# Moving the low parts of activations and weights from VectorE to GpSimd in a two-layer feed-forward

## The chip, the cores and the metric

The kernel runs on one core of one Trainium2 chip. The metric is the device time of one execution in microseconds (us). TensorE has two clock levels here, 1.2 and 2.4 GHz, and the profile records which one was granted.

## The reference, cut to what matters

A delta-rule attention (batch 4, 8 heads, 768 steps, head size 48) makes x of 3072 tokens by 384 features. Two feed-forward layers follow:

```
_moe_ref:  h = x @ w_in                              # 384 -> 2048
           P = a[0] + a[1]*h + a[2]*h^2 + a[3]*h^3
           Q = 1.0 + |b[0]|*|h| + |b[1]|*h^2
           g = P / (Q + 1e-06)                       # the rational layer, layer 0
           x = g @ w_out                             # 2048 -> 384
_moe2_ref: h = x @ w_in;  sp = log(1 + exp(h));  g = h * tanh(sp)   # layer 1
           out = g @ w_out
```

## The kernel before

**Stages.** `delta_rule` runs first, in six tiles of 512 tokens (T = 6, TOK = 512). Its GpSimd program inverts small triangular matrices (lines 224 and 227, tiles `inv_t` and `inv_x`), while VectorE keeps the recurrence going. Then `feed_forward` runs layer 0 over six tiles and layer 1 over six tiles. In its original form GpSimd has no program in `feed_forward`.

**Products in three parts.** A float32 product is made of three fp32r matmuls: high x high, high x low, low x high. So each operand is kept as a high part (a rounded copy, made by ScalarE) and a low part (the operand minus its high part, made by VectorE). Tokens: `x_raw` to `x_hi` (line 918) and `x_lo` (line 1041). Weights: `w_raw` to `w_hi` (line 83) and `w_lo` (line 87). Each such part of x or of one weight pair has 128x1536 elements. Two parities of `x_hi` and `x_lo` and two buffers of `w_raw` exist; `x_raw` is single, and its next load waits for `x_lo_ready`. The load of weight pair n waits until the low part of pair n - 2 is made.

**Blocks.** The 2048 hidden features are cut into 8 pairs of 128 (NP = 8). One block is one pair of one tile: 18 matmuls into `h_ps`, the elementwise function on 128x1024 elements, and 18 matmuls into `o_ps`. `two_tiles` covers 16 blocks (DT = 16), so each layer has 48. TensorE issues the first product of block n + 2 and then the second product of block n. ScalarE's order in a layer-0 block is: square, abs and linear term of block n + 1 (885 to 887), `g_hi` of block n (895), logarithm and exponential of block n + 1 (906, 914), which give the reciprocal. VectorE's order is

```
1018 ratio      val <- val, rec        1026 corrected  den <- den, rec
1031 corrected  val <- den, val         991 below      den <- sq, den
1037 low_part   g_lo <- val, g_hi       997 above      pa  <- pa, h_ps
 999 above      val <- pa, h_ps
```

Lines 997 and 999 read one tile in SBUF and one in PSUM; the other five read two tiles in SBUF. Layer 1 has six VectorE operations in a block: 1020, 1004 (a clip with one input), 1028, 1031, 1010 (reads `h_ps`) and 1037.

**Where the low parts stand.** Splits of x are written into the order by hand. ScalarE makes `x_hi` behind its work of n = 2 and n = 10, and VectorE makes `x_lo` behind its work of n = 3 and n = 11, that is, behind line 999 of that block. The lists LATE and SWAP place the weights: LATE names pairs 4 to 7 of layer 0, in its first blocks; SWAP names the eight pairs of layer 1 (numbers 8 to 15), in the last blocks of layer 0 and the first ones of layer 1. ScalarE makes `w_hi` at the end of the block before the one in which VectorE makes `w_lo`. Pairs 0 to 3 are prepared within `delta_rule`.

Of the kernel before, what the change touches and what calls it, by code (L numbers as in the profile page):

```python
# [5 lines left out]
F32 = mybir.dt.float32  # L6
F32R = mybir.dt.float32r
ALU = mybir.AluOpType
# [7 lines left out]
T = S // (C * CT)  # L16
# [13 lines left out]
NP = FT // 2  # L30
# [8 lines left out]
LATE = [(0, i, i - NP // 2 + 1) for i in range(NP // 2, NP)]  # L39
SWAP = [(1, i, NP + 3 + i) for i in range(NP)]  # L40
# [696 lines left out]
def feed_forward(nc, x1, x2, w1, w2, coef, out, w, hand):  # L737
# [3 lines left out]
    with ExitStack() as ctx:  # L741
        def sb(name, shape, dt=F32):
            return ctx.enter_context(nc.sbuf_tensor(name, shape, dt))

        def sem(name):
            return ctx.enter_context(nc.semaphore(name))

        x_raw = hand.x_raw
        x_hi = sb("x_hi", [P, 2, KT, TOK], F32R)
        x_lo = sb("x_lo", [P, 2, KT, TOK], F32R)  # L750
# [15 lines left out]
        x_hi_ready, x_lo_ready = sem("x_hi_ready"), sem("x_lo_ready")  # L766
# [12 lines left out]
        DT = 2 * NP  # L779
        block = ctx.enter_context(nc.Block())  # L780

        def features(t):
            return t.rearrange("(k p) n -> p k n", p=P)

        @block.sync
        def _(sp):
            def load_x(src, t, tile):

                sp.wait_ge(x_lo_ready, tile)
                hand.load_x(sp, src, t)  # L790

            def store(dst, t, tile):
                sp.wait_ge(o_copied, tile + 2)
                sp.dma_start(features(dst[:, t]), o_stage).then_inc(o_stored, 16)

            sp.dma_start(cf[:, 0:6], coef).then_inc(coef_loaded, 16)

            for cp in range(2):
                sp.wait_ge(hand.y_stored[cp], 32 * T + 32)
            load_x(x1, 1, 1)  # L800
            for i in range(NP // 2 + 2, NP):
                w.load(sp, w1, i)
            with sp.Fori(0, T - 2) as t:
                store(x2, t, t)
                load_x(x1, t + 2, t + 2)
            store(x2, T - 2, T - 2)

            sp.wait_ge(o_stored, 16 * 2)
            load_x(x2, 0, T)
            for i in range(NP):  # L810
                w.load(sp, w2, NP + i)
            store(x2, T - 1, T - 1)
            sp.wait_ge(o_stored, 16 * (T + 1))
            load_x(x2, 1, T + 1)
            with sp.Fori(0, T - 2) as t:
                store(out, t, t + T)
                load_x(x2, t + 2, t + T + 2)
            store(out, T - 2, 2 * T - 2)
            store(out, T - 1, 2 * T - 1)
            sp.wait_ge(o_stored, 16 * (2 * T + 1))  # L820
# [56 lines left out]
        def _(act):  # L877
# [48 lines left out]
            def copy_out(tile):  # L926

                act.wait_ge(g_used, NP * tile + NP + 2)

                act.wait_ge(o_stored, 16 * tile + 16)  # L930
                act_fn(o_stage, o_ps[:], ACT.Copy).then_inc(o_copied, 1)  # L931
# [48 lines left out]
            two_tiles(1, T - 1, None)  # L980
            copy_out(2 * T - 1)

        @block.vector
        def _(dve):
            dve_tt, dve_stt = nc.vector.tensor_tensor, nc.vector.scalar_tensor_tensor

            def below(dt, n):

                e = n % 2
                dve.wait_ge(abs_ready, DT * dt + n + 1)  # L990
                dve_stt(den[:, e], sq[:, e], cf[:, 6:7], den[:, e], ALU.mult, ALU.add).then_inc(q_ready, 1)  # L991

            def above(dt, n):

                e = n % 2
                dve.wait_ge(lead_ready, DT * dt + n + 1)
                dve_tt(pa[:, e], pa[:, e], h_ps[e][:], ALU.mult).then_inc(inner_ready, 1)  # L997
                dve.wait_ge(inner_ready, DT * dt + n + 1)
                dve_stt(val[:, e], pa[:, e], cf[:, 1:2], h_ps[e][:], ALU.add, ALU.mult).then_inc(h_read, 1)  # L999

            def clipped(dt, n):
                e = n % 2
                dve.wait_ge(exp_ready, DT * dt + n - NL1 + 1)
                nc.vector.tensor_scalar(den[:, e], den[:, e], EXP20, None, ALU.min).then_inc(clip_ready, 1)

            def mish_above(dt, n):

                e = n % 2
                dve.wait_ge(one_ready, DT * dt + n - NL1 + 1)
                dve_stt(val[:, e], sq[:, e], -1.0, h_ps[e][:], ALU.add, ALU.mult).then_inc(h_read, 1)  # L1010

            def ratio(layer, dt, n):

                e = n % 2
                dve.wait_ge(rec_ready, DT * dt + n + 1)
                dve.wait_ge(h_read, DT * dt + n + 1 + 2)
                if layer == 0:
                    dve_stt(val[:, e], val[:, e], cf[:, 0:1], rec[:, e], ALU.add, ALU.mult).then_inc(ratio_ready, 1)  # L1018
                else:
                    dve_tt(val[:, e], val[:, e], rec[:, e], ALU.mult).then_inc(ratio_ready, 1)  # L1020

            def corrected(layer, dt, n):

                e = n % 2
                if layer == 0:
                    dve_stt(den[:, e], den[:, e], ONE, rec[:, e], ALU.add, ALU.mult).then_inc(unit_ready, 1)  # L1026
                else:
                    dve_stt(den[:, e], sq[:, e], 1.0, rec[:, e], ALU.add, ALU.mult).then_inc(unit_ready, 1)
                dve.wait_ge(ratio_ready, DT * dt + n + 1)
                dve.wait_ge(unit_ready, DT * dt + n + 1)  # L1030
                dve_stt(val[:, e], den[:, e], 2.0, val[:, e], ALU.subtract, ALU.mult).then_inc(g_ready, 1)  # L1031

            def low_part(dt, n):

                e = n % 2
                dve.wait_ge(g_hi_ready, DT * dt + n + 1)
                dve_stt(g_lo[:, e], val[:, e], -1.0, g_hi[:, e].bitcast(F32), ALU.mult, ALU.subtract).then_inc(g_lo_ready, 1)  # L1037

            def split(tile, par):
                dve.wait_ge(x_hi_ready, tile + 1)  # L1040
                dve_tt(x_lo[:, par], x_raw[:], x_hi[:, par].bitcast(F32), ALU.subtract).then_inc(x_lo_ready, 1)

            def two_tiles(layer, dt, after, splits=()):

                for n in range(DT):
                    following = layer if n + 1 < DT else after
                    ratio(layer, dt, n)
                    if following == 1:
                        clipped(dt, n + 1)
                    corrected(layer, dt, n)  # L1050
                    if following == 0:
                        below(dt, n + 1)
                        low_part(dt, n)
                        above(dt, n + 1)
                    elif following == 1:
                        mish_above(dt, n + 1)
                        low_part(dt, n)
                    else:
                        low_part(dt, n)
                    if n == 3:  # L1060
                        split(2 * dt + 1, 1)
                    if n == NP + 3 and after is not None:
                        split(2 * dt + 2, 0)
                    for l, i, at in splits:
                        if at == n:
                            w.split_lo(nc, dve, NP * l + i)

            dve.sem_inc(g_used, 2)
            dve.sem_inc(h_read, 2)
            nc.vector.memset(shifts[:, 0:1], ONE)  # L1070
            nc.vector.memset(shifts[:, 1:2], 1.0).then_inc(coef_made, 1)
            split(0, 0)
            dve.wait_ge(coef_made, 2)
            below(0, 0)
            above(0, 0)
            two_tiles(0, 0, 0, LATE)
            with dve.Fori(1, T // 2 - 1) as dt:
                two_tiles(0, dt, 0)
            two_tiles(0, T // 2 - 1, 1, [x for x in SWAP if x[2] < DT])
            two_tiles(1, T // 2, 1, [(l, i, n - DT) for l, i, n in SWAP if n >= DT])  # L1080
            with dve.Fori(T // 2 + 1, T - 1) as dt:
                two_tiles(1, dt, 1)
            two_tiles(1, T - 1, None)
# [49 lines left out]
```

## Time and profile before

| what | value |
|---|---|
| median of 3 runs | 1302.22 us (1290.46 to 1315.64) |
| the profiled execution, time | 1274.1 us |
| its span, first to last instruction | 1272.0 us |
| mean granted TensorE clock | 0.932 |
| busy: PE, DVE, ACT, POOL | 1148.9, 932.5, 740.7, 194.8 us |

The profile calls TensorE PE, VectorE DVE, ScalarE ACT and GpSimd POOL. Its times are microseconds from the start of the span. The profiled execution lies below the three timed ones, so sums are made within its span and then carried over to the median as a difference.

### The profile page before, as it was taken

How to read it: one execution, taken by the hardware profiler on the slowest of the kernel's cores; microseconds unless marked ns; L12 is line 12 of the kernel's file. 1: busy time of each engine (PE TensorE's matmuls, PEld its weight loads, DVE VectorE, ACT ScalarE, POOL GpSimd, SP SyncE). 2: the span in 40 equal slices, each digit the busy share in tenths (PEclk: the TensorE clock that was granted, in tenths of full speed). 3: DMA queues.
4: the chain of work that ended last, by engine and by line, in shares of the span. 5: the costliest groups of instructions: out<-in, count | busy, mean ns of one | idle time of the engine just before them, and what ended most of it. 6: DMA issues, size and time to landing. Idle time of an engine off the chain costs nothing.

```text
span 1272.0 us, 23564 instructions
## 1 busy us (share of the span) xinstructions
PE 1148.9 (90%) x9612; PEld 885.4 (70%) x9612; DVE 932.5 (73%) x1042; ACT 740.7 (58%) x932; POOL 194.8 (15%) x365
## 2 busy tenths in 40 slices
PE   6169797979999888999999999988999999999997
PEld 3147474657666666777878777776888888888885
DVE  2733343434444599999999999999978787878885
ACT  1123242424343676777777786878776666667664
POOL 1508655565810000000000000000000000000000
PEclk7569797959899999999999999999999999999999
DMA  6985665645371210101010010223010100001000
GB/s 143 197 166 119 141 142 151 133 111 143 77 206 41 62 50 1 50 1 50 0 46 4 0 50 1 99 67 107 26 50 1 46 4 26 24 12 38 1 26 25
DMA packets 81694, 83.82 MB, mean 66 GB/s; under 512 B 55040, under 2 KB 62720, under 8 KB 81024
## 3 DMA queue, kind: packets, MB, share of 16 engines
q1 hardware_dynamic: 70880, 60.43, 19.0%
q10 hardware_dynamic: 10720, 22.03, 6.3%
q8 instruction: 73, 1.20, 0.4%
q14 instruction: 21, 0.17, 0.0%
HBM read 61.99 MB, written 20.45 MB: 65 GB/s over the span
## 4 chain that ended last, share of the span: by engine, by line
PE 34%; DVE 25%; ACT 4%; issue 3%; DMA 0%; DVEq 0%; ACTq 0%
PE o_ps L825 6%; PE o_ps L826 6%; PE o_ps L827 6%; PE h_ps L825 5%; PE h_ps L827 5%; PE h_ps L826 5%; DVE val L999 4%; DVE val L1018 4%; DVE val L1031 4%; DVE g_lo L1037 3%; DVE den L991 3%; DVE den L1026 3%; DVE pa L997 3%; ACT stage L931 1%; ACT den L886 1%
## 5 line engine op out<-in xcount | busy, mean ns | idle before, releaser
L895 ACT ACTIVATE g_hi<-val 128x1024 fp32r<-128x1024 f32 x96 | 102.0, 1062 | 89.5 <-DVE val L1031 83.7
L825 PE MATMUL o_ps<-g_hi,w_hi_early 128*128 128x512 f32 x288 | 116.6, 405 | 17.8 <-ACT stage L931 14.2
L681 DVE TENSOR_TENSOR u_blk<-hz_ps,w_blk 128x768 f32<-128x768 f32 x48 | 46.0, 957 | 115.5 <-PE hz_ps L390 115.5
L825 PE MATMUL o_ps<-g_hi,w_hi_late 128*128 128x512 f32 x288 | 115.6, 401 | 15.6 <-DVE g_lo L1037 15.6
L1031 DVE SCALAR_TENSOR_TENSOR val<-den,val 128x1024 f32<-128x1024 f32 x96 | 117.7, 1226 | 10.7 <-DVE den L1026 0.5
L525 ACT ACTIVATE stage<-y_ps 128x256 f32<-128x256 f32 x48 | 18.2, 380 | 178.9 <-PE y_ps L422 178.5
L1037 DVE SCALAR_TENSOR_TENSOR g_lo<-val,g_hi 128x1024 fp32r<-128x1024 f32 x96 | 117.6, 1225 | 3.7 <-ACT g_hi L895 3.4
L826 PE MATMUL o_ps<-g_lo,w_hi_early 128*128 128x512 f32 x288 | 115.2, 400 | 0.0
L825 PE MATMUL h_ps<-x_hi,w_hi_early 128*128 128x512 f32 x288 | 113.0, 392 | 2.4 <-DVE val L999 2.0
L827 PE MATMUL o_ps<-g_hi,w_lo_early 128*128 128x512 f32 x288 | 115.0, 399 | 0.0
L825 PE MATMUL h_ps<-x_hi,w_hi_late 128*128 128x512 f32 x288 | 112.5, 391 | 1.6 <-DVE w_lo_late L87 1.6
L826 PE MATMUL o_ps<-g_lo,w_hi_late 128*128 128x512 f32 x288 | 113.0, 392 | 0.0
L827 PE MATMUL o_ps<-g_hi,w_lo_late 128*128 128x512 f32 x288 | 112.8, 392 | 0.0
L826 PE MATMUL h_ps<-x_lo,w_hi_early 128*128 128x512 f32 x288 | 112.8, 392 | 0.0
L827 PE MATMUL h_ps<-x_hi,w_lo_early 128*128 128x512 f32 x288 | 112.6, 391 | 0.0
L826 PE MATMUL h_ps<-x_lo,w_hi_late 128*128 128x512 f32 x288 | 112.1, 389 | 0.0
L827 PE MATMUL h_ps<-x_hi,w_lo_late 128*128 128x512 f32 x288 | 112.1, 389 | 0.0
L367 PE MATMUL warm_ps<-eye 128*128 128x512 bf16 x348 | 110.8, 417 | 0.0
L914 ACT ACTIVATE rec<-rec 128x1024 f32<-128x1024 f32 x96 | 101.0, 1052 | 1.5
L227 POOL TENSOR_TENSOR inv_x<-inv_x,inv_t 128x112 f32<-128x112 f32 (+18 forms) x177 | 97.1, 549 | 13.9
L224 POOL TENSOR_TENSOR inv_t<-inv_n,inv_x 128x112 f32<-128x112 f32 (+18 forms) x177 | 87.7, 496 | 64.2 <-DMA inv_n<-n_dram 50.8
L889 ACT ACTIVATE den<-h_ps 128x1024 f32<-128x1024 f32 x48 | 49.3, 1026 | 67.2 <-PE h_ps L827 67.2
(96 smaller groups left out, 2367.0 us busy)
## 6 DMA issues: line engine op xcount, KB each, us to landing
w_raw<-w SPq DMA_DIRECT2D x14, 768.0 KB, 4.3
kq_gram<-kq_t SPq DMA_DIRECT2D x12, 768.0 KB, 11.1
x_raw<-x_dram SPq DMA_DIRECT2D x12, 768.0 KB, 5.6
kq_run<-kq_t ACTq DMA_DIRECT2D x40, 192.0 KB, 4.0
kv_run<-kv_n ACTq DMA_DIRECT2D x20, 384.0 KB, 5.4
k_norm<-kv_n SPq DMA_DIRECT2D x6, 768.0 KB, 4.9
x_dram<-stage ACTq DMA_DIRECT2D x24, 192.0 KB, 5.1
x_dram<-stage SPq DMA_DIRECT2D x6, 768.0 KB, 4.1
```

The lines of the kernel that those rows point to most:

```text
L224: tt(inv_t[:, 0:r, c], inv_n[:, 0:r, r:r + 1].broadcast_to(shape), inv_x[:, r:r + 1, c].broadcast_to(shape), ALU.mult).then_inc(step, 1)
L227: tt(inv_x[:, 0:r, c], inv_x[:, 0:r, c], inv_t[:, 0:r, c], ALU.subtract).then_inc(step, 1)
L367: nc.tensor.matmul(warm_ps[:], operand[:, 0:P], operand, start=True, stop=True)
L825: nc.tensor.matmul(dst, hi, rhs_hi, start=first, stop=False)
L826: nc.tensor.matmul(dst, hi, rhs_lo, start=False, stop=False)
L827: return nc.tensor.matmul(dst, lo, rhs_hi, start=False, stop=last)
L895: act_fn(g_hi[:, n % 2], val[:, n % 2], ACT.Copy, scale=-1.0).then_inc(g_hi_ready, 1)
L914: act_fn(rec[:, e], rec[:, e], ACT.Exp, scale=-1.0).then_inc(rec_ready, 1)
L999: dve_stt(val[:, e], pa[:, e], cf[:, 1:2], h_ps[e][:], ALU.add, ALU.mult).then_inc(h_read, 1)
L1018: dve_stt(val[:, e], val[:, e], cf[:, 0:1], rec[:, e], ALU.add, ALU.mult).then_inc(ratio_ready, 1)
L1031: dve_stt(val[:, e], den[:, e], 2.0, val[:, e], ALU.subtract, ALU.mult).then_inc(g_ready, 1)
L1037: dve_stt(g_lo[:, e], val[:, e], -1.0, g_hi[:, e].bitcast(F32), ALU.mult, ALU.subtract).then_inc(g_lo_ready, 1)
```

## The change

GpSimd gets a program in `feed_forward`. It makes `x_lo` of tiles 1 to 6 (all of layer 0 but the first tile, and the first tile of layer 1) and `w_lo` of pairs 4 to 15, each as soon as ScalarE has signalled the high part. VectorE keeps `x_lo` of tile 0 and of tiles 7 to 11, and loses the twelve weight splits and six x splits from its order. Nothing else moves.

```
+        @block.gpsimd
+        def _(pool):
+            def split(tile):
+                pool.wait_ge(x_lo_ready, tile)
+                pool.wait_ge(x_hi_ready, tile + 1)
+                nc.gpsimd.tensor_tensor(x_lo[:, tile % 2], x_raw[:], x_hi[:, tile % 2].bitcast(F32),
+                                        ALU.subtract).then_inc(x_lo_ready, 1)
+
+            def split_w(n):
+                pool.wait_ge(w.lo_ready, n)
+                pool.wait_ge(w.hi_ready, n + 1)
+                nc.gpsimd.tensor_tensor(w.lo[n % NP], w.raw[:, n % 2], w.hi[n % NP].bitcast(F32),
+                                        ALU.subtract).then_inc(w.lo_ready, 1)
+
+            split_w(NP // 2)
+            split_w(NP // 2 + 1)
+            split(1)
+            for n in range(NP // 2 + 2, NP):
+                split_w(n)
+            for tile in range(2, T + 1):
+                split(tile)
+            for n in range(NP, 2 * NP):
+                split_w(n)
...
-            def two_tiles(layer, dt, after, splits=()):
+            def two_tiles(layer, dt, after):
...
-                    if n == 3:
+                    if layer and n == 3:
                         split(2 * dt + 1, 1)
-                    if n == NP + 3 and after is not None:
+                    if layer and n == NP + 3 and after is not None:
                         split(2 * dt + 2, 0)
-                    for l, i, at in splits:
-                        if at == n:
-                            w.split_lo(nc, dve, NP * l + i)
...
-            two_tiles(0, 0, 0, LATE)
+            two_tiles(0, 0, 0)
...
-            two_tiles(0, T // 2 - 1, 1, [x for x in SWAP if x[2] < DT])
-            two_tiles(1, T // 2, 1, [(l, i, n - DT) for l, i, n in SWAP if n >= DT])
+            two_tiles(0, T // 2 - 1, 1)
+            two_tiles(1, T // 2, 1)
```

## Rows read from the trace of the kernel before

**Rows 1.** The page, the span in 40 equal slices, busy tenths.

```profile
PE   6169797979999888999999999988999999999997
DVE  2733343434444599999999999999978787878885
POOL 1508655565810000000000000000000000000000
```

**Rows 2.** Stretches: span, busy us (count) of PE, PEld, DVE, ACT, POOL; clock, DMA, GB/s.

```profile
560.00:820.00 260.00, 246.80 (x1039) 197.95 (x1039) 250.52 (x209) 193.71 (x183) 0.00 (x0) 0.97 0.09 31
1000.00:1200.00 200.00, 200.00 (x884) 165.58 (x884) 165.87 (x151) 139.06 (x129) 0.00 (x0) 1.00 0.07 24
```

**Rows 3.** Timeline of VectorE, layer 0: start, duration, line, operation.

```profile
537.48 1.29 DVE L1018 SCALAR_TENSOR_TENSOR val<-val,cf,rec 128x1024 f32<-128x1024 f32 x1
...
543.50 1.21 DVE L997 TENSOR_TENSOR pa<-pa,h_ps 128x1024 f32<-128x1024 f32 x1
544.75 1.28 DVE L999 SCALAR_TENSOR_TENSOR val<-pa,cf,h_ps 128x1024 f32<-128x1024 f32 x1
545.95 1.75 DVE L1041 TENSOR_TENSOR x_lo<-x_raw,x_hi 128x1536 fp32r<-128x1536 f32 x1
547.62 1.28 DVE L1018 SCALAR_TENSOR_TENSOR val<-val,cf,rec 128x1024 f32<-128x1024 f32 x1
...
556.28 1.29 DVE L1018 SCALAR_TENSOR_TENSOR val<-val,cf,rec 128x1024 f32<-128x1024 f32 x1
```

**Rows 4.** Timeline of VectorE: first and last block start around LATE and SWAP splits.

```profile
442.79 1.28 DVE L1018 SCALAR_TENSOR_TENSOR val<-val,cf,rec 128x1024 f32<-128x1024 f32 x1
...
485.01 1.27 DVE L1018 SCALAR_TENSOR_TENSOR val<-val,cf,rec 128x1024 f32<-128x1024 f32 x1
...
823.35 1.28 DVE L1018 SCALAR_TENSOR_TENSOR val<-val,cf,rec 128x1024 f32<-128x1024 f32 x1
...
865.73 1.28 DVE L1018 SCALAR_TENSOR_TENSOR val<-val,cf,rec 128x1024 f32<-128x1024 f32 x1
```

**Rows 5.** Timeline of VectorE, first blocks of layer 1 with weight splits.

```profile
874.02 1.22 DVE L1020 TENSOR_TENSOR val<-val,rec 128x1024 f32<-128x1024 f32 x1
...
880.58 1.75 DVE L87 TENSOR_TENSOR w_lo_late<-w_raw,w_hi_late 128x1536 fp32r<-128x1536 f32 x1
882.25 1.22 DVE L1020 TENSOR_TENSOR val<-val,rec 128x1024 f32<-128x1024 f32 x1
```

**Rows 6.** Timeline of ScalarE: one weight and one x high part.

```profile
449.93 1.47 ACT L83 ACTIVATE w_hi_late<-w_raw 128x1536 fp32r<-128x1536 f32 x1
...
535.69 1.47 ACT L918 ACTIVATE x_hi<-x_raw 128x1536 fp32r<-128x1536 f32 x1
```

**Rows 7.** Groups by shape on GpSimd: busy us, mean ns, idle before.

```profile
L227 POOL TENSOR_TENSOR inv_x<-inv_x,inv_t 128x255 f32<-128x255 f32 x10 | 7.4, 736 | 0.8
...
L227 POOL TENSOR_TENSOR inv_x<-inv_x,inv_t 128x31 f32<-128x31 f32 x10 | 2.7, 273 | 0.8
...
L333 POOL COPY inv_x<-eye 128x1024 f32<-128x1024 f32 x1 | 1.0, 1037 | 14.8 <-DMA eye<-consts 14.8
```

**Rows 8.** Timelines of GpSimd and VectorE: a long VectorE operation is there first.

```profile
342.47 1.77 DVE L87 TENSOR_TENSOR w_lo_early<-w_raw,w_hi_early 128x1536 fp32r<-128x1536 f32 x1
```

**Rows 9.** Timeline of GpSimd: the same line and shape, earlier and beside it.

```profile
324.73 0.59 POOL L224 TENSOR_TENSOR inv_t<-inv_n,inv_x 128x220 f32<-128x220 f32 x1
...
342.71 1.97 POOL L224 TENSOR_TENSOR inv_t<-inv_n,inv_x 128x220 f32<-128x220 f32 x1
```

**Rows 10.** Timelines: VectorE's L627 with GpSimd idle, then beside a GpSimd operation.

```profile
74.08 0.29 DVE L627 TENSOR_TENSOR w_blk<-w_next,blk_mask 128x128 f32<-128x128 f32 x1
...
322.61 0.58 POOL L227 TENSOR_TENSOR inv_x<-inv_x,inv_t 128x192 f32<-128x192 f32 x1
322.69 0.66 DVE L627 TENSOR_TENSOR w_blk<-w_next,blk_mask 128x128 f32<-128x128 f32 x1
```

**Rows 11.** Timeline of TensorE at the start of a tile's second products.

```profile
662.42 0.54 PE L825 MATMUL o_ps<-g_hi,w_hi_early 128*128 128x512 f32 x1 [2.66 <-ACT stage L931]
662.76 0.63 PE L826 MATMUL o_ps<-g_lo,w_hi_early 128*128 128x512 f32 x1
...
664.89 0.63 PE L825 MATMUL o_ps<-g_hi,w_hi_early 128*128 128x512 f32 x1
```

## The prediction

> **What bounds the kernel now.** I read the page's 40 slices first. The change acts only in the feed-forward, which is the right-hand two thirds: VectorE stands at 9 tenths from slice 15 to 28 (layer 0), and at 7 to 8 in layer 1, where TensorE stands at 9; GpSimd is empty from slice 14 on [rows 1]. The stretches say the same in microseconds. In 260 us of layer 0 VectorE is busy 250.5; in 200 us of layer 1 TensorE is busy all 200 and VectorE 165.9 [rows 2]. So in layer 0 VectorE sets the pace and in layer 1 TensorE does, and the timeline of VectorE must give the price of a split. From one line 1018 to the next takes 10.14 us with an `x_lo` in between (537.48 to 547.62) and 8.66 us without (547.62 to 556.28) [rows 3]: the split of 1.75 us costs 1.48 us net, since an operation overlaps the next a little and a small gap before line 1018 vanishes. TensorE's own pace is a little shorter than either. In 200 us of layer 1 it started 884 matmuls, 0.226 us each, and a block has 36: 8.15 us [rows 2]. In layer 0 it has therefore only about 0.5 us of slack in a block.
>
> **What leaves VectorE, in layer 0.** The LATE stretch runs over four blocks from 442.79 to 485.01, 42.22 us, with five splits (four weight pairs and x tile 1); four plain blocks would take 34.64, so these cost 7.58 us. The SWAP stretch from 823.35 to 865.73, 42.38 us, has again four blocks and five splits (x tile 6, pairs 8 to 11): 7.74 us [rows 4]. The x tiles 2 to 5 cost 4 x 1.48 = 5.9 us. The sum is 21.2 us for 14 splits. The remaining four, pairs 12 to 15, stand in the first blocks of layer 1 on VectorE. There a block with a split takes 8.23 us (874.02 to 882.25) [rows 5], which is TensorE's pace, so taking them away is worth about nothing; I put 0 to 0.5 us for the four. If GpSimd's work were free, the whole gain would be **21 us, 1.6%**.
>
> **What is added on GpSimd.** No operation of 1536 elements stands in GpSimd's trace. From the same line and kind with two inputs, 31 elements take 273 ns and 255 take 736 ns [rows 7]: 2.07 ns an element and about 0.2 us fixed. That makes 1536 x 2.07 + 0.2 = 3.4 us. The lower end is GpSimd's copy with one input, 1037 ns for 1024, about 0.8 ns an element over the same fixed part [rows 7]: 1.5 us. The type written is fp32r here and f32 there; for that I find no row, and VectorE's row of 1.75 us for the same split [rows 3] only bounds from another engine. I take 3.3 us, near the rows with two inputs, which were themselves measured in part beside VectorE. In GpSimd's own queue there is nothing to delay: the splits come a block or more apart, and only where x and a weight come together (tiles 1 and 6) do two stand behind each other, some 7 us. TensorE needs none of them before two blocks or more have gone by, so its waits for them stay at nothing. `x_raw` and `w_raw` come free at about the same time as before, and the loads wait on the same counts, on SP's queue as before.
>
> **What it does to VectorE.** This is the term that decides. At 342.47 VectorE begins its own weight split, two inputs in SBUF. GpSimd's operation begins at 342.71 and takes 1.97 us [rows 8, 9]; the same line and shape took 0.59 at 324.73 [rows 9]. It ended 0.44 us after VectorE's did: it had waited for the whole of it. The other way round, GpSimd begins at 322.61, VectorE's line 627 at 322.69, and this takes 0.66 us where it takes 0.29 with GpSimd idle [rows 10]: it waited 0.37 us, until about 0.1 us before GpSimd's operation was over. So the two engines exclude each other when both read two tiles in SBUF, for about a whole operation, and whoever is there first goes first. Five of layer 0's seven VectorE operations are of that kind.
>
> Now the place. `x_hi` ends at 537.16 [rows 6]; GpSimd would begin at about 537.20, and VectorE's next operation with two SBUF inputs at 537.48 [rows 3]. GpSimd is first, holds until 537.20 + 3.3 - 0.1 = 540.4, and line 1018 starts 2.9 us late. `w_hi` of pair 5 ends at 451.40 [rows 6], and line 1018 would start, without the split, at about 451.47: 3.1 to 3.2 us late. The pattern repeats at every split of layer 0. ScalarE signals just as lines 997 and 999, which read PSUM, end; so their 2.45 us (543.50 to 545.95) [rows 3], the only cover in the block, lie behind it.
>
> The Trainium skill (SBUF — State Buffer, section "SBUF: two separate sides") goes further than the rows. It says that VectorE and GpSimd share one pair of ports under an exclusive lock, held for the whole instruction, and that VectorE wants it in two-port modes or with two SBUF inputs. The rows of 1.97 and 0.66 us agree [rows 9, 10]; by that rule the sum comes out as below, without it at -21 us. Its page on GpSimd (GPSIMD Engine Reference, § Reconciling with measured numbers) gives 4497 ns for a tensor_tensor of 2048 elements; scaled, that would be an estimate of 3.4 us here and change nothing.
>
> **The sum.** In layer 0 fifteen GpSimd operations fall: x tiles 1 to 6 and pairs 4 to 12, since pair 12's high part is made one block before the layer ends. 6 x 2.9 + 9 x 3.15 = 45.8 us of standing, against 21.2 saved: +24.6. In layer 1 pairs 13 to 15 remain. A block there needs 8.23 - 1.67 = 6.56 us of VectorE without the split [rows 5]; with a stall of 3.1 it is 9.7 against TensorE's 8.15, so +1.5 each, +4.6 together. Then TensorE. At a tile's start it sits idle 2.66 us and its next matmuls are 0.43 us apart instead of 0.23 (durations 0.63) [rows 11], the lower clock level. A stall of 3 us gives it a similar gap. Some eight matmuls are then 0.2 us longer apart, 1.6 us, of which the block's slack of 0.5 takes a part at once; so that costs between 0 and 1.1 us a stall, 0 to 16 us for fifteen. Since TensorE works a block ahead of VectorE, I take a value near the lower end, 2 us. Together **+31 us**, with 0.9 us less or more a stall as GpSimd's operation is shorter or longer by that. The profiled execution would go from 1274.1 to about 1305 us, the median from 1302 to **1333 us, +2.4%**.
>
> **The rivals.** *No effect on VectorE* (chance 0.13): long operations could share where short ones wait, or GpSimd could give way each time. All splits then run in VectorE's shadow: -21 us, 1281 us. Rows 9 speak against it. *GpSimd comes last* (0.17): when it waits, VectorE's next operation, already queued, is let in before it, and it gets its turn only beside lines 997 and 999. Then a split costs 3.2 - 2.45 = 0.75 us, fifteen of them 11 us against 21.2, plus about 1 us in layer 1: -9 us, 1293 us. For it: VectorE's operations overlap by 0.1 us and leave hardly a gap. Against: GpSimd's signal comes before line 1018 starts, so it doesn't have to wait. *The end on the other side of no change* is the forecast itself reversed by these two; the point at which the sign turns is a stall of 1.4 us a split. *A slow GpSimd subtract into fp32r* (0.06): if the type written costs it twice the time, the stall is 6 us, fifteen are 90, and with layer 1 the sum is about +80 us. *The edit does nothing that counts* (within 5 us of now, 0.02) would need VectorE not to be the bound in layer 0, against rows 2. The forecast keeps 0.62.
>
> **How the numbers follow.** The forecast's own range is from a stall of 2.4 us (+17) to one of 3.3 with most of the clock's toll (+45), that is 1319 to 1347 us; the three runs before spread by 12 us to either side, which widens the ends a little. The range of 8 in 10 takes in the second rival and leaves out most of the first and the slow subtract: 1284 to 1352. A difference below about 2% can't be told from no change here, 26 us. Of the forecast's 0.62 I count 0.46 above that and 0.16 below, of the others 0.07 above (the slow subtract, and scatter), and 0.05 of the first rival reaches below -2%. That gives 0.05 faster, 0.42 within, 0.53 slower.
>
> **What would show it.** VectorE's line 1018 (or its next operation with two SBUF inputs) behind each `x_hi` or `w_hi` should read near 4.2 us instead of 1.28, the block with it 11.6 instead of 10.14, and GpSimd's eighteen subtracts near 3.3 us. The clock record should show more drops in layer 0. Lines 997 and 999 should keep their durations, also beside GpSimd. Blocks of layer 0 without a split should stay at 8.66 us. I would be wrong if line 1018 kept 1.28 us beside a GpSimd subtract, or if the subtracts were stretched instead, to 4.5 us and more, and ended beside line 999.

## The result and the profile after

The changed kernel takes 1322.97 us in the median of 6 runs (1313.05 to 1342.67), the kernel before 1295.73 us in 6 runs (1281.72 to 1315.64). The ratio of these two medians is 1.021. The executions of a kernel fall into a faster and a slower group, the profiled one of the change (1342.67 us) is of the slower, and the ratio that counts is taken over the faster ones alone: 1.032, 95% interval 1.025 to 1.039. A second comparison (below, `change_again`) gives 1.023, 1.017 to 1.030. So the change makes the kernel some 2 to 3% slower; 1333 us and +2.4% had been predicted.

The whole time is a blunt tool here. The stage before the feed-forward, in which nothing was changed, lasts between 420 and 457 us in the twelve profiles of this study, as more or less of it runs at TensorE's lower clock level (its mean granted clock is 0.83 of full speed in the 420 us and 0.73 in the 457), and the profile of the change happens to have its longest one. So I read every profile by its **feed-forward stretch**, from ScalarE's first `x_hi` to the end of the span. These are the starts of that stretch before and after, and its three parts: until VectorE's first ratio operation, layer 0, and from the first ratio of layer 1 to the end. First the kernel before (window; PE, PEld, DVE, ACT, POOL busy; clock; DMA; GB/s):

```profile
420.07 1.49 ACT L918 ACTIVATE x_hi<-x_raw 128x1536 fp32r<-128x1536 f32 x1 [1.42 <-PEq L112]
...
420.07:433.91 13.84, 11.44 (x49) 8.77 (x49) 5.54 (x6) 8.59 (x9) 0.00 (x0) 1.00 0.27 79
433.91:874.02 440.11, 408.57 (x1717) 326.14 (x1718) 426.25 (x350) 329.69 (x309) 0.00 (x0) 0.98 0.10 33
874.02:1272.00 397.98, 388.88 (x1705) 320.52 (x1703) 324.92 (x295) 270.56 (x250) 0.00 (x0) 0.99 0.09 28
```

and the changed one:

```profile
456.90 1.49 ACT L918 ACTIVATE x_hi<-x_raw 128x1536 fp32r<-128x1536 f32 x1 [1.42 <-PEq L112]
...
456.90:470.74 13.84, 11.44 (x49) 8.77 (x49) 5.55 (x6) 8.59 (x9) 0.00 (x0) 1.00 0.26 79
470.74:935.50 464.76, 412.37 (x1710) 328.64 (x1710) 450.54 (x336) 328.28 (x308) 66.12 (x15) 0.97 0.10 33
935.50:1340.70 405.20, 390.80 (x1710) 321.67 (x1710) 327.88 (x292) 272.17 (x251) 10.49 (x3) 0.99 0.08 26
```

The stretch grew from 851.9 to 883.8 us: nothing at the start, +24.7 in layer 0, +7.2 in layer 1, **+31.9** in all. How well such a stretch repeats is known from two kernels that were profiled twice: 883.8 and 885.8 us for the change, 837.8 and 837.9 for `shared` below. The kernel before has one profile, so a difference from it of 2 us or less says little. VectorE has 15 splits less in layer 0 (the counts in the rows differ by 14, because 336 takes in layer 1's first ratio at the edge) and is yet busy 24 us longer. The timeline shows on which operations. Here VectorE, ScalarE and GpSimd around x tile 2; in the changed kernel line 1042 is the ratio (1018 before), 1050 and 1055 are the corrections (1026, 1031), 1021 and 1023 the two that read PSUM (997, 999):

```profile
579.60 1.22 DVE L1021 TENSOR_TENSOR pa<-pa,h_ps 128x1024 f32<-128x1024 f32 x1
...
580.71 1.47 ACT L918 ACTIVATE x_hi<-x_raw 128x1536 fp32r<-128x1536 f32 x1
580.85 1.28 DVE L1023 SCALAR_TENSOR_TENSOR val<-pa,cf,h_ps 128x1024 f32<-128x1024 f32 x1
...
582.24 1.28 DVE L1042 SCALAR_TENSOR_TENSOR val<-val,cf,rec 128x1024 f32<-128x1024 f32 x1
582.32 4.57 POOL L988 TENSOR_TENSOR x_lo<-x_raw,x_hi 128x1536 fp32r<-128x1536 f32 x1 [59.46 <-ACT x_hi L918]
...
583.45 4.53 DVE L1050 SCALAR_TENSOR_TENSOR den<-den,rec 128x1024 f32<-128x1024 f32 x1
...
588.09 1.23 DVE L1055 SCALAR_TENSOR_TENSOR val<-den,val 128x1024 f32<-128x1024 f32 x1
...
594.22 1.28 DVE L1042 SCALAR_TENSOR_TENSOR val<-val,cf,rec 128x1024 f32<-128x1024 f32 x1
```

The reader is to see two waits, neither of them marked as idle time, because both engines were given their instructions and count as busy. GpSimd's subtract begins 0.08 us after line 1042 and lasts 4.57 us, 1.1 of which it waits for that operation. Line 1050 then lasts 4.53 us instead of 1.22 (1.22 is what the same line takes in the blocks without a split): it waits 3.3 us for GpSimd. From ratio to ratio it is 11.98 us, where a block with VectorE's own split takes 10.14 and one without 8.66 [rows 3]. In layer 0 fifteen VectorE operations are longer in this way, by 2.8 to 3.3 us each, 48.5 us together.

In layer 1 it is the clip that waits, an operation with a single input, both in SBUF:

```profile
936.78 3.48 POOL L994 TENSOR_TENSOR w_lo_late<-w_raw,w_hi_late 128x1536 fp32r<-128x1536 f32 x1 [6.58 <-ACT w_hi_late L83]
948.17 3.50 POOL L994 TENSOR_TENSOR w_lo_late<-w_raw,w_hi_late 128x1536 fp32r<-128x1536 f32 x1 [7.91 <-ACT w_hi_late L83]
```

```profile
937.58 3.24 DVE L1028 TENSOR_SCALAR den<-den 128x1024 f32<-128x1024 f32 x1 [0.87 <-ACT den L889]
...
948.98 3.25 DVE L1028 TENSOR_SCALAR den<-den 128x1024 f32<-128x1024 f32 x1 [2.21 <-ACT den L889]
```

These two GpSimd subtracts found VectorE out of the way and give the length of one alone: 3.5 us. The clip takes 0.69 us elsewhere in this layer, so it waits 2.6.

### The profile page after: what moved, and what is told of

Its sections match the earlier page's. It is cut to its first block, busy times and chain, and to the rows that moved or that the text cites. A ratio compares the mean times of both kernels' runs of the same rounds, so it can differ in the third digit from the quotient of the medians.

```text
span 1340.7 us, 23582 instructions
## 1 busy us (share of the span) xinstructions
PE 1195.0 (89%) x9612; PEld 916.6 (68%) x9612; DVE 960.8 (72%) x1024; ACT 740.7 (55%) x932; POOL 271.4 (20%) x383
## 4 chain that ended last, share of the span: by engine, by line
DVE 34%; PE 28%; ACT 2%; issue 1%; DVEq 0%; ACTq 0%
DVE den L1050 6%; DVE val L1055 5%; PE o_ps L825 5%; PE o_ps L827 5%; PE o_ps L826 5%; PE h_ps L825 5%; PE h_ps L827 5%; PE h_ps L826 5%; DVE val L1042 5%; DVE val L1023 4%; DVE den L1015 4%; DVE g_lo L1061 4%; DVE pa L1021 4%; DVE den L1028 1%; DVE den L1052 0%
## 5 line engine op out<-in xcount | busy, mean ns | idle before, releaser
L1055 DVE SCALAR_TENSOR_TENSOR val<-den,val 128x1024 f32<-128x1024 f32 x96 | 123.9, 1290 | 10.3
L367 PE MATMUL warm_ps<-eye 128*128 128x512 bf16 x348 | 123.7, 459 | 0.0
L825 PEld LDWEIGHTS o_ps<-g_hi,w_hi_early 128*128 128x128 f32 x288 | 56.5, 196 | 58.8 <-DVE g_lo L1061 30.0
```

What stands on the lines that cost most here:

```text
L367: nc.tensor.matmul(warm_ps[:], operand[:, 0:P], operand, start=True, stop=True)
L825: nc.tensor.matmul(dst, hi, rhs_hi, start=first, stop=False)
```

## The experiments

All are changes of one of the two kernels, with the code cut to what matters, read by the feed-forward stretch; 851.9 us is before, 883.8 the change.

**x alone, and weights alone.** `x_only` gives the weights' low parts back to VectorE, `w_only` those of x.

```
 x_only: pool:  for tile in range(1, T + 1): split(tile)        # no split_w
         dve:   LATE and SWAP splits as before
 w_only: pool:  for n in range(NP // 2, 2 * NP): split_w(n)     # no split
         dve:   split(2 * dt + 1, 1), split(2 * dt + 2, 0) as before, in both layers
```

> GpSimd makes only the x low parts of tiles 1 to 6; VectorE makes all weight low parts again. I read the feed-forward stretch, from ScalarE's first x_hi to the end of the span: 851.9 us before, 883.8 after the change. Exclusion (each GpSimd subtract stops VectorE for about 3.3 us in place of a split of 1.48): six times 1.8, so 863 us, and VectorE's operations beside the subtracts last 4.5 us. Rival, that the weights' low parts now come late and TensorE waits for them: x alone costs nothing or gains, 843 to 852 us.

> GpSimd makes only the low parts of the weight pairs 4 to 15; VectorE makes all x low parts again. Exclusion: nine stalls of 3.3 us in layer 0 against 12 us of splits saved, and three of 1.5 net in layer 1: +22, so 874 us in the feed-forward stretch. Rival, x parts on GpSimd are what costs: 840 to 852 us. The two changes should add up to the whole one (+32) within 2 us if each operation pays for itself.

Measured: 860.4 us (+8.5) and 874.1 us (+22.2); together +30.7 against +31.9 for the whole change. So the parts add up. In layer 0 six x subtracts cost 8.4 us and nine of weights 15.0, 1.4 and 1.7 us each; the +7.2 of layer 1 is all in `w_only` (+7.2 there, +0.2 in `x_only`). The stalled operation stands behind a subtract of either kind; this is `w_only`, pair 5 (its ratio is line 1033, the correction behind it 1041):

```profile
459.53 1.28 DVE L1033 SCALAR_TENSOR_TENSOR val<-val,cf,rec 128x1024 f32<-128x1024 f32 x1
459.61 4.57 POOL L988 TENSOR_TENSOR w_lo_late<-w_raw,w_hi_late 128x1536 fp32r<-128x1536 f32 x1 [14.74 <-ACT w_hi_late L83]
460.73 4.53 DVE L1041 SCALAR_TENSOR_TENSOR den<-den,rec 128x1024 f32<-128x1024 f32 x1
```

**GpSimd at work, nothing handed over.** The kernel before, with an extra GpSimd operation at the same eighteen moments, for which nobody waits.

```
+            def extra(done, n):
+                pool.wait_ge(done, n + 1)          # w.hi_ready or x_hi_ready, as in the change
+                nc.gpsimd.tensor_tensor(spare[:], spare[:], spare[:], ALU.subtract).then_inc(spare_set, 1)
...             # extra_none_in: three nc.gpsimd.memset(spare[:], 0.0) in its place
```

> The kernel before with one GpSimd operation added at each of the eighteen places, two inputs of 128x1480 in a spare tile; nobody waits for it. VectorE still makes every low part, so nothing comes later or from another engine. Exclusion: fifteen stalls of 3.2 us in layer 0 and three with about 1.5 to 3 us net in layer 1: +52 to +57, so 904 to 909 us in the feed-forward stretch. Rival, the change costs through handing over the low parts (late parts, more semaphores) and not through a stop of VectorE: 852 us.

> The same places, but three memsets of 128x1480 each in a row (about 3.9 us together): GpSimd writes SBUF and reads nothing. If what the two engines share is taken by any GpSimd operation: stalls as with two inputs, +50 us or more, about 905 us. If only a GpSimd operation that reads SBUF stops VectorE, as the page SBUF, State Buffer, of the Trainium skill says for VectorE's two-input operations: 852 us, or a little over it through VectorE's clip with one input in layer 1.

The subtract costs 894.8 us (+42.9) though every low part is still made by VectorE at its old place. Three memsets, longer together (4.13 us), cost 853.4 (+1.5). So the rival, that handing over is what costs, falls, and so does the thought that any work on GpSimd would do it in layer 0: the memsets only write SBUF, the subtract reads it too. A GpSimd operation with one input was not run. The sum was below what I expected, since this subtract held VectorE for 2.45 us and not 3.2 (line 1049 below is the first correction; `forms` asks why). In `extra_two_in`:

```profile
567.28 1.28 DVE L1041 SCALAR_TENSOR_TENSOR val<-val,cf,rec 128x1024 f32<-128x1024 f32 x1
567.36 3.71 POOL L989 TENSOR_TENSOR spare<-spare 128x1480 f32<-128x1480 f32 x1 [63.78 <-ACT x_hi L920]
568.48 3.67 DVE L1049 SCALAR_TENSOR_TENSOR den<-den,rec 128x1024 f32<-128x1024 f32 x1
```

and in `extra_none_in`, first a place in layer 0, where a memset runs beside operations with two SBUF inputs, then one of the three in layer 1 where a clip is longer (1.76, 1.08 and 1.77 us):

```profile
559.55 1.22 DVE L1053 SCALAR_TENSOR_TENSOR den<-den,rec 128x1024 f32<-128x1024 f32 x1
559.83 2.73 POOL L990 MEMSET spare<- 128x1480 f32 x2
560.89 1.23 DVE L1058 SCALAR_TENSOR_TENSOR val<-den,val 128x1024 f32<-128x1024 f32 x1
...
894.43 4.55 POOL L990 MEMSET spare<- 128x1480 f32 x3 [4.75 <-ACT w_hi_late L83]
894.81 1.22 DVE L1047 TENSOR_TENSOR val<-val,rec 128x1024 f32<-128x1024 f32 x1
895.95 1.76 DVE L1031 TENSOR_SCALAR den<-den 128x1024 f32<-128x1024 f32 x1
```

A VectorE operation with two SBUF inputs keeps its time beside a memset; the clip, one input and one output in SBUF, waits 1.1 us for it. The page SBUF — State Buffer of the Trainium skill (section "SBUF: two separate sides") makes just this difference: VectorE's operations in a two-port mode exclude any GpSimd operation, those with two SBUF inputs only one that reads SBUF. The trace agrees, 1.22 against 1.76 us, though it doesn't mark in which mode the clip runs.

**The same work in another place.** `in_window` leaves all eighteen subtracts on GpSimd, but lets each wait until VectorE has finished `g_lo` of a block, which is when VectorE starts its two operations on PSUM (with x tile 1 moved to block 5, so that pairs 6 and 7 come first).

```
             def split_w(n, block):
+                pool.wait_ge(g_lo_ready, block + 1)
                 pool.wait_ge(w.lo_ready, n)
...
+            for _, i, at in LATE: split_w(i, at)
+            split(1, 5)
+            for tile in range(2, T + 1): split(tile, NP * (tile - 1) + 3)
+            for _, i, at in SWAP: split_w(NP + i, NL1 - DT + at)
```

> All eighteen subtracts on GpSimd as in the change, but each waits for g_lo of a block, so that it begins together with the two VectorE operations that read PSUM (lines 997 and 999, 2.45 us). Exclusion of operations with two SBUF inputs only: a stall of about 1 us instead of 3.3 in layer 0 (4.3 where x tile 6 and pair 8 come together), 3.3 in layer 1, where line 1020 comes next: about 853 us in the feed-forward stretch, the same time as before within 1%. Rival, GpSimd stops any VectorE operation: as with the change, 880 us or more.

Measured: 849.4 us in the stretch, 34 less than the change with the same instructions on the same engines; the ratio to the kernel before is 0.992 (0.987 to 0.998). At x tile 2 the stall is down to 0.83 us:

```profile
573.59 1.22 DVE L1021 TENSOR_TENSOR pa<-pa,h_ps 128x1024 f32<-128x1024 f32 x1
...
573.75 3.51 POOL L989 TENSOR_TENSOR x_lo<-x_raw,x_hi 128x1536 fp32r<-128x1536 f32 x1 [49.95 <-DVE g_lo L1061]
574.84 1.28 DVE L1023 SCALAR_TENSOR_TENSOR val<-pa,cf,h_ps 128x1024 f32<-128x1024 f32 x1
...
576.24 2.11 DVE L1042 SCALAR_TENSOR_TENSOR val<-val,cf,rec 128x1024 f32<-128x1024 f32 x1
```

Lines 1021 and 1023 run beside GpSimd at their plain durations, so operations that read one tile in SBUF and one in PSUM don't wait. The other stalls of layer 0 are 0.8 to 0.85 us too, but for one of 3.3 us where pair 8's subtract follows that of x tile 6. Layer 0 takes 430.7 us, 9.5 less than before. Layer 1 takes 405.0 us, 7.0 more: there the subtract still runs into the clip.

```profile
899.88 3.04 DVE L1028 TENSOR_SCALAR den<-den 128x1024 f32<-128x1024 f32 x1 [0.88 <-ACT den L889]
```

So in layer 0 the place alone turns the sign, from +24.7 to -9.5: what GpSimd does under those 2.45 us costs VectorE nothing, and what it does beside operations with two SBUF inputs VectorE waits for.

**Pieces that fit.** `x_halves` cuts the x split into two pieces of 768 columns, each beside the PSUM operations of one of two successive blocks, for tiles 1 to 5; the rest is VectorE's as before. `shared` does this for tiles 2 to 5 and gives GpSimd the first 896 columns of pairs 4 to 11, VectorE the other 640.

```
+            def piece(tile, block, k, done):        # k: columns
+                pool.wait_ge(g_lo_ready, block + 1)
+                pool.wait_ge(x_hi_ready, tile + 1)
...
+                piece(tile, at, slice(0, half), False)
+                piece(tile, at + 1, slice(half, 2 * half), True)
...
+                nc.gpsimd.tensor_tensor(w.lo[n % NP][:, 0:WCUT], w.raw[:, n % 2, 0:WCUT],     # shared
+                                        w.hi[n % NP][:, 0:WCUT].bitcast(F32), ALU.subtract).then_inc(w_part, 1)
```

> The x low parts of tiles 1 to 5 on GpSimd in two pieces of 768 columns, each begun with VectorE's PSUM operations of two successive blocks; everything else on VectorE as before. A piece takes 0.2 + 768 x 2.1 ns = 1.8 us and fits under 2.45. Exclusion: no stall, five splits of 1.48 us gained, 844.5 us in the feed-forward stretch, 0.6% faster in all. Rival, that the handover or a fixed cost per GpSimd operation stays: 852 us or more.

> GpSimd makes the x low parts of tiles 2 to 5 in two pieces as in x_halves, and the first 896 columns of the weight pairs 4 to 11 beside the PSUM operations; VectorE makes the other 640 columns and all the rest. Exclusion: 4 x 1.48 + 8 x 0.9 = 13 us gained, 839 us in the feed-forward stretch, 1% faster. If windows are missed, stalls show on line 1018 and the stretch is 852 or more.

Measured: 843.7 us (-8.2) and 837.8 us (-14.1), with no VectorE operation of a block above its plain duration in layer 0. Two rows of `shared`, GpSimd's part of a weight and VectorE's:

```profile
458.75 2.14 POOL L1000 TENSOR_TENSOR w_lo_late<-w_raw,w_hi_late 128x896 fp32r<-128x896 f32 x1 [90.09 <-DVE g_lo L1068]
...
461.03 0.82 DVE L88 TENSOR_TENSOR w_lo_late<-w_raw,w_hi_late 128x640 fp32r<-128x640 f32 x1
461.77 1.28 DVE L1049 SCALAR_TENSOR_TENSOR val<-val,cf,rec 128x1024 f32<-128x1024 f32 x1
```

The whole time of `x_halves` has a ratio of 0.989 (0.979 to 0.999, from 4 runs), which leaves nearly no change possible. The first timing of `shared` (median 1292.29 us of 10 runs against 1296.02 of 19) gave no ratio with an interval, so it was timed again.

> The same kernel as shared, timed once more against the kernel before: 839 of 852 us in the feed-forward stretch is 14 of 1290 us, a ratio of 0.989. What scatters is the stage before the feed-forward, so the interval should hold 0.989 and may reach 1.

The ratio is 0.991, interval 0.986 to 0.996, and the stretch again 837.9 us. This version is 0.9% faster than the kernel before, and its stretch is 46 us shorter than that of the change.

**The change again.**

> The change once more against the kernel before on the same chip. If the feed-forward stretch is all that differs, 32 of 1290 us, the ratio is 1.025 and the stretch again 884 us; if something outside it is slower too, the ratio stays at 1.032 or above and the stage before the feed-forward is longer than in the other runs (420 to 453 us) in most of them.

The ratio is 1.023 (1.017 to 1.030), the stretch 885.8 us, and the stage before it 424.1 us. So the change's own cost is 32 to 34 us, about 2.5%. What the first comparison showed above that I can't place: it isn't in the stretch, and of the change's two profiles one has the longest stage before it (457 us) and one nearly the shortest (424). Both intervals hold 1.025.

**What sets GpSimd's length.**

> The kernel before with eighteen short extra GpSimd subtracts in three kinds, six of each: two different inputs written back as f32 (490 columns), the same input twice written back as f32 (480), two different inputs written as fp32r (490). It asks why the extra operation of 1480 columns held VectorE for only 2.4 us where the real split of 1536 held it for 3.3. If the type written costs GpSimd time, the fp32r kind is 0.2 to 0.3 us longer than the other two, about 1.27 against 1.0 us at the shortest. If a second, different input costs it, the first and third kind agree at about 1.27 and the one with the same input is at about 1.0.

The stretch was 862.8 us. An operation's length depends on what VectorE does when it starts, so only equal places can be compared. There the fp32r and the f32 kind with two inputs are equal, 2.12 and 2.12 us behind an x tile, 2.39 and 2.39 behind a weight: the type written is free. The kind with the same input twice is hardly shorter at the same places: 2.05 us behind an x tile, 2.33 behind a weight, and 1.31 against 1.37 in the first blocks of layer 1.

```profile
620.63 2.05 POOL L995 TENSOR_TENSOR spare<-spare 128x480 f32<-128x480 f32 x1 [69.94 <-ACT x_hi L921]
692.27 2.12 POOL L995 TENSOR_TENSOR spare_r<-spare 128x490 fp32r<-128x490 f32 x1 [69.59 <-ACT x_hi L921]
763.99 2.12 POOL L995 TENSOR_TENSOR spare<-spare 128x490 f32<-128x490 f32 x1 [69.60 <-ACT x_hi L921]
```

The shortest ones seem to say more, 0.99 us (480 columns) with the same input twice and 1.17 (490, fp32r) with two. But the latter began at 901.37, while VectorE's line 1049 (900.41 to 901.63) was still at work, and the operation of 1480 columns that began at the same point in `extra_two_in` took 2.77 us instead of its 2.65 out of VectorE's way. So I estimate from these rows, ten columns allowed for, that a second, different input costs about 0.05 us at 490 columns, and three times that at 1480. The gap to explain is about 0.7 us (2.65 us, against some 3.4 when 3.5 is scaled to 1480 columns). Neither the type written nor the second input accounts for it. In the real split the two inputs lie in two tiles of their own, here in two halves of one tile; whether that matters was not tried, and the cause stays open.

## Why the prediction was right, step by step

**VectorE sets the pace of layer 0, TensorE that of layer 1; a split is worth 1.48 us.** Right. Blocks without a split stayed at 8.68 us (530.19 to 538.87 in the changed kernel), and `x_halves`, which takes five splits away at no price, gained 8.2 us where 5 x 1.48 = 7.4 were due.

**GpSimd's subtract takes 3.3 us.** It takes 3.5 alone. The working had given 3.4 from the rows of the delta rule [rows 7], and I went below it without a row for that. The open point, whether fp32r costs time, came out as no.

**The two exclude each other, and GpSimd stops VectorE for about its length.** Right, and it is the whole result: `extra_two_in` shows the stop without any handing over, `in_window` shows it down to 0.85 us a split in layer 0 with all of the handing over. Expected were fifteen stalls of 2.9 to 3.15 us in layer 0, 45.8 us; there are fifteen with 48.5.

**GpSimd comes first, so line 1018 waits.** Wrong in the detail. ScalarE's signal reaches GpSimd 0.14 us after `x_hi` ends (580.71 + 1.47 = 582.18, begin 582.32), where I had allowed 0.04, and `x_hi` also ended a little later than before; in most places the ratio is already running, GpSimd waits for it, and the correction behind it stands. It changed nothing in the sum: whoever loses the first turn, VectorE loses GpSimd's length once. It is also why GpSimd's rows read 4.57 us, a length that I had named as a sign of being wrong: it is 3.5 us and a wait of 1.1, and it ends beside line 1050, not beside the two that read PSUM. The second rival had built on the same race and supposed that VectorE's next operation, queued already, would be let in before the waiting GpSimd. It isn't: at 583.45 line 1050 overlaps its predecessor and still waits.

**The sum of layer 0** was +24.6 and came to +24.7. Two errors cancel. The stalls are 2.7 us more. The part measured ends at layer 1's first ratio, and pair 12's split on VectorE (872.36, 1.67 us net) lay within it, which I had counted as worth nothing; about 1 us more came back, as VectorE's waits for `g_hi` at the tile starts became shorter (2.3 to 1.1 us in sum). That last part is chance: in the change's second profile they are 2.4 us, and layer 0 takes 466.8 us, +26.7. So that the sum was met to 0.1 us is luck. That it was met to some 2 us in both profiles is not.

**Layer 1** was put at +4.6 and cost +7.2, in both profiles. The step that failed is the cover: I had let TensorE's slack take up half of each stall. The three stalls are 2.6 us each (3.25 - 0.69), and they fall on the clip. VectorE already waits for ScalarE's exponential ahead of the clip (0.87 us at 937.58), and I had left this wait out: 6.56 + 0.87 + 2.56 = 9.99 us, where the block took 10.05; with the wait of 2.21 us the next one comes to 11.33, and took 11.41. Nor is this wait slack that could take up the stall, since ScalarE in turn waits for the clip:

```profile
940.85 1.16 ACT L900 ACTIVATE sq<-den,shifts 128x1024 f32<-128x1024 f32 x1 [3.30 <-DVE den L1028]
...
947.93 1.01 ACT L889 ACTIVATE den<-h_ps 128x1024 f32<-128x1024 f32 x1
```

It makes the next exponential (line 889) only behind this, so a late clip makes the next one late. That an operation with one input would wait for GpSimd I had not considered; the trace of the delta rule before had shown it, where VectorE's copies of 32 columns grew from 0.17 to 0.57 us beside GpSimd.

**TensorE's clock** was to cost 2 us. In layer 0 the clock record has ten drops to the lower level instead of six, and in most blocks no time is seen to come from them: the block with a stalled split is 11.98 us, which is 8.66 + 3.32. The second profile shows that they can cost something. There TensorE, after 2.73 us without work at a tile's start, runs at the lower level, 1.2 GHz, from 605 to 611.3 us (granted clock 0.50 of full speed), ScalarE's next square then waits 4.20 us for `h_ps` instead of 2.87 in the first profile, and that block takes 11.00 us instead of 9.68. So the clock cost 1.3 us more there than in the first profile, of the size that I had put in. From the second profile:

```profile
605.00:611.30 6.30, 6.16 (x15) 4.87 (x16) 6.07 (x7) 5.25 (x7) 0.00 (x0) 0.50 0.75 250
...
616.55 1.03 ACT L885 ACTIVATE sq<-h_ps 128x1024 f32<-128x1024 f32 x1 [4.20 <-PE h_ps L827]
```

**The whole** was +31 us and is +31.9 in the stretch (+33.9 in the second profile). The interval of the first comparison begins at 2.5%, a little above the 2.4% given.

**The rivals.** No effect on VectorE (-21 us) falls with line 1050 at 4.53 us. GpSimd last (-9 us) falls with the same row. A slow subtract into fp32r falls with 3.5 us and with `forms`. An edit that does nothing that counts falls with the ratio's interval, 1.017 at its lowest.

## What to carry to other kernels

Work moved from a bound VectorE to GpSimd isn't free because GpSimd is idle: if GpSimd reads SBUF and VectorE's operations read two tiles there, they take turns, and GpSimd needs twice as long for the same subtract (3.5 against 1.75 us). In these runs it paid only beside VectorE operations that read PSUM, cut to fit under them and started by a semaphore that VectorE raises there. Look for it in a trace as operations that last longer than their group's plain duration, not as idle time. Before counting on an engine's idle time to cover a stall, look at what that idle time waits for: in layer 1 it was an engine that itself waited for the stalled operation.

## What the runs showed of the hardware

VectorE with two SBUF inputs against a GpSimd subtract with two: a wait until it is over (4.53 instead of 1.22 us), also where VectorE's operation was queued right behind the one before it. The same against a GpSimd memset: no wait (1.22 and 1.23 us). VectorE's clip with one SBUF input and SBUF output: 1.76 us against a memset and 3.25 against a subtract, instead of 0.69. VectorE with one SBUF and one PSUM input against a GpSimd subtract: no wait (1.22 and 1.28 us). GpSimd's split of 1536, 896 and 768 columns took 3.5, 2.14 and 1.86 us where nothing was in its way: 2.1 to 2.2 us for every further 1000 columns.
